# Twenty-two more identity products on TensorE in the first units of a fused attention, soft-MoE and squared-ReLU kernel

## The reference, cut to what matters

```python
# q, k, v: (8, 8, 576, 64); pool = 8, so 72 pooled keys per head
k_p = k.reshape(B, H, Sp, pool, D).mean(axis=3)
v_p = v.reshape(B, H, Sp, pool, D).mean(axis=3)
scores = scale * np.matmul(q, k_p.transpose(0, 1, 3, 2))
attn = softmax(scores)                      # over the 72 keys
x = (attn @ v_p) rearranged to (4608, 512)
logits = x @ phi                            # 32 slots
slot_out = per expert: relu((softmax(logits, 0).T @ x) @ w1) @ w2
x = softmax(logits, 1) @ slot_out
h = maximum(x @ w_in, 0);  out = (s * h * h + b) @ w_out
```

## Time and profile before

| | |
|---|---|
| median of 3 runs | 648.23 us |
| profiled execution | 652.14 us, span 650.3 us |
| busy in the span | PE 97%, DVE 74%, ACT 69%, POOL 19% |
| mean granted clock of PE | 0.986 of full speed |
| HBM | 70.32 MB read, 9.44 MB written |

### The profile page before, as it was taken

The page is one execution under the profiler, slowest core; times in us unless marked ns, Lnnn a source line. Parts: engine busy times, 40 slices in busy tenths (PEclk is TensorE's granted clock), DMA queues, the critical chain, the costliest instruction groups (busy, mean ns, idle before and its releaser), DMA issues.

```text
span 650.3 us, 16686 instructions
## 1 busy us (share of the span) xinstructions
PE 629.7 (97%) x6462; PEld 547.8 (84%) x6462; DVE 481.5 (74%) x796; ACT 448.9 (69%) x754; POOL 124.2 (19%) x126
## 2 busy tenths in 40 slices
PE   7799999999999999999999999999999999999996
PEld 7676776776763347889999999999999999999996
DVE  4888665665535739886888878888888887888876
ACT  1588766676522169996777777777777777777772
POOL 3787887542210010004000000000000000000001
PEclk9699989999999999999999999999999999999999
DMA  9968879386459980001000000000000000000001
GB/s 330 321 196 328 331 236 404 77 329 250 158 206 411 414 366 1 1 1 42 26 34 18 34 16 32 16 32 16 32 16 30 18 32 16 16 32 16 33 18 66
DMA packets 26005, 80.50 MB, mean 124 GB/s; under 512 B 6496, under 2 KB 14688, under 8 KB 23392
## 3 DMA queue, kind: packets, MB, share of 16 engines
q1 hardware_dynamic: 25952, 79.76, 32.9%
HBM read 70.32 MB, written 9.44 MB: 123 GB/s over the span
## 4 chain that ended last, share of the span: by engine, by line
PE 89%; DVE 3%; DMA 2%; POOL 2%; issue 2%; ACT 1%; DVEq 0%; ACTq 0%; POOLq 0%
PE bank L1999 16%; PE bank L2010 16%; PE bank L2000 16%; PE bank L1904 5%; PE bank L1772 5%; PE bank L1725 2%; PE bank L1751 2%; PE bank L1927 2%; PE bank L1631 2%; PE bank L1934 2%; PE bank L1930 2%; PE bank L1864 2%; PE bank L1840 2%; PE bank L1663 2%; DMA kvbuf<-in_v_dram 2%
## 5 line engine op out<-in xcount | busy, mean ns | idle before, releaser
L1388 DVE TENSOR_TENSOR lo_sb<-a_sb,hi_sb 128x896 fp32r<-128x896 f32 x128 | 140.1, 1094 | 57.2 <-PE bank L2010 55.5
L1053 ACT ACTIVATE hi_sb<-a_sb 128x896 fp32r<-128x896 f32 x128 | 122.2, 955 | 77.1 <-PE bank L2000 74.8
L1999 PE MATMUL bank<-w_hi,hi_sb 128*128 128x256 f32 x381 | 96.9, 283 | 0.0
L2000 PE MATMUL bank<-w_lo,hi_sb 128*128 128x256 f32 x381 | 96.9, 283 | 0.0
L1038 ACT ACTIVATE a_sb<-r_sb 128x512 f32<-128x512 f32 x144 | 91.1, 632 | 6.4
L2010 PE MATMUL bank<-w_hi,lo_sb 128*128 128x256 f32 x381 | 87.1, 283 | 0.0
L1031 ACT ACTIVATE r_sb<-bank 128x512 f32<-128x512 f32 x144 | 83.6, 580 | 0.1
L1999 PEld LDWEIGHTS bank<-w_hi,hi_sb 128*128 128x128 f32 x381 | 73.2, 192 | 0.0
L2000 PEld LDWEIGHTS bank<-w_lo,hi_sb 128*128 128x128 f32 x381 | 73.2, 192 | 0.0
L864 POOL TENSOR_TENSOR pu_sb<-pu_sb,logits 128x256 f32<-128x256 f32 x1 | 0.7, 740 | 334.5 <-DVE x_sb L1446 334.5
L1999 PE MATMUL bank<-t_early,hi_sb 128*128 128x256 f32 x256 | 64.3, 283 | 0.0
(11 more groups left out here) (213 smaller groups left out, 1333.0 us busy)
## 6 DMA issues: line engine op xcount, KB each, us to landing
early_third<-in_moe_w_dram SPq DMA_DIRECT2D x5, 2048.0 KB, 11.5
kvbuf<-in_k_dram SPq DMA_DIRECT2D x12, 768.0 KB, 5.6
kvbuf<-in_v_dram SPq DMA_DIRECT2D x12, 768.0 KB, 6.1
out_dram<-o_sb SPq DMA_DIRECT2D x36, 256.0 KB, 2.3
qbuf<-in_q_dram SPq DMA_DIRECT2D x8, 1024.0 KB, 7.9
early<-in_moe_w_dram SPq DMA_DIRECT2D x4, 2048.0 KB, 9.9
late<-in_moe_w_dram SPq DMA_DIRECT2D x3, 2048.0 KB, 14.3
after_last<-in_moe_w_dram SPq DMA_DIRECT2D x2, 2048.0 KB, 8.2
```

Source lines behind the costliest of these rows:

```text
L1053: act.activation(hi_sb[:, n % 2, :], a_sb[:, n % ARING, P:2 * CH], ACT.Copy).then_inc(hi_ready, 1)
L1388: dve.tensor_tensor(lo_sb[:, n % 2, :], a_sb[:, n % ARING, P:2 * CH], hi_sb[:, n % 2, :].bitcast(F32), ALU.subtract).then_inc(lo_ready, 1)
L1999: pe.matmul(acc, hi, rhs_hi, start=(k == 0 and (at == AT1 or at % 2 == 1)), stop=False, skip_group_check=True)
L2000: last = pe.matmul(acc, hi, rhs_lo, start=False, stop=False, skip_group_check=True)
```

## The change

`START_WARM` becomes four numbers in place of one. The first stands where the 7 products stood, behind the turn of the first keys. The others stand in steps 0, 1 and 2 of PE's loop, behind the turn of the queries (and in step 0 behind the turns of keys). 7 become 12 + 3 + 10 + 4 = 29.

```diff
-    START_WARM = 7
+    START_WARM = (12, 3, 10, 4)
...
             turn_keys(0, 0, 0)
-            for _ in range(START_WARM):
-                pe.matmul(bank[A_B[0]][:, 0:P], ident[:, :], ident[:, :], start=True, stop=True)
+            def fill_start(times):
+                for _ in range(times):
+                    pe.matmul(bank[A_B[0]][:, 0:P], ident[:, :], ident[:, :], start=True, stop=True)
+
+            fill_start(START_WARM[0])
...
                 if n == 0:
                     turn_keys(0, 1, 0)
                     turn_keys(0, 2, 0)
+                if n < GP:
+                    fill_start(START_WARM[1 + n])
```

## The result

The changed kernel is slower. Its median is 651.75 us over twelve executions on the chip, that of before 648.02 us over twelve beside it; the ratio is 1.0051, with a 95% interval of 1.003 to 1.0071, so it loses 3.3 us (2 to 4.6). I had forecast 646.4 us, 0.3% faster.

A forecast was written before the change was run, and what follows sets the result against it. PE, busy for 97% of the span, was taken as the bound; a full clock in front was to bring the chain's 50.78 us to 48.95, 1.8 us off the median of 648.23: 646.4 us, range 644.5 to 648.3.

The forecast's parts named there:

- What bounds the kernel, and the clock: PE, busy 97% of the span; filling its early holes should keep the clock full past 14.5 us, to about 21.
- The products themselves cost nothing: Front of PE's order: the 22 added products fit in existing waits at no cost; uncovered, 5.5 us at full clock.
- The gain at the load of values: DVE's first key group of the second pair starts at 26.15 us; SP's load of values leaves at 31.65, not 33.50.
- The sum: 50.78 becomes 48.95, 1.8 us less.: Chain's turn of weights on PE comes 1.8 us earlier, own range 1.2 to 2.3; forecast with both clock variants 62%.
- the four groups that each ends in "nothing": Behind first keys 5 products, before first scores 3, first values 10, second values 4: each said to cost nothing.
- the first rival: Late clock fall near 89.5 us moves: gone, 644.7 us (10%), or one more fall or instruction wait, 648.1 us (12%).
- The half clock: Third rival: clock half through the ten and four products in front, 1.9 us slower, 650.1 us; 8%.
- The late fall of the clock: Half clock from about 89.5 to 93 us disappears, gaining 1.7 us more, 3.5 in all: 644.7 us; 10%.

The follow-up runs named there:

- thin: Changed kernel with its 22 added products only one column wide, the first 7 kept: same instructions, next to no array work; 653.91 us, ratio 1.0085.
- held loads: Two 2 MB loads held until the queries of unit 30 are turned: ratio 0.9971 in the kernel before, 0.9995 changed, 0.9958 in the wide one, 1.0011 thin.
- the changed kernel run again: The changed kernel measured once more without any edit, beside the kernel before: 651.77 us, ratio 1.0048.
- the wide one: Changed kernel's front work as products of up to 512 columns, 4 instructions more than the kernel before instead of 88: 647.05 us, ratio 0.9991.
- The four comparisons at an equal place of the code: Warm against cold front at the same or 4 instructions' different code place: 0.09% and 0.34 to 0.37% with loads unmoved, 0.13% and 0.16% with them held.
- the displaced kernels: Kernels with 88 instructions more than before, changed and thin: ratios 1.0051, 1.0048 and 1.0085; with the two loads held 0.9995 and 1.0011.
- the held kernel before: The kernel before with only the two 2 MB loads held back: 646.20 us, ratio 0.9971.
- all four kernels of the table: Before, the wide one, changed and thin, each without and with held loads: ratios 1, 0.9991, 1.0051 and 1.0048, 1.0085; held 0.9971, 0.9958, 0.9995, 1.0011.

## Why the prediction was wrong

*What bounds the kernel, and the clock.* Right. The clock stayed full from before 9 us on; the fall at 14.5 and the return at 28 us are gone, in all eight profiles with the work of 29 products in front. What I did not see is that the cold stretch of before is not the same in every execution: two profiles with a cold front have it for 13.7 us (before, thin), two for 6.8 (both with held loads).

*The products themselves cost nothing.* Right as to the array: the first three groups ended before what stood behind them was released (11.9 against 12.62, 18.4 against 18.84 us), and the fourth ran up to the turn of values at 21.65, behind which the scores waited 0.24 us for DVE anyway.

*The gain at the load of values.* Right in mechanism and size: I had the first group of keys at 26.15 behind its load, it was at 26.00; the load of values at 31.65, it left at 31.46; the chain at 48.95, it was 49.20. PE has a new wait of 0.88 us for its own instructions at 40.6 on this chain; in the changed kernel run again it is missing, and the turn begins at 48.53.

*"The sum: 50.78 becomes 48.95, 1.8 us less."* This is the step that failed, and with it the line of the four groups that each ends in "nothing". I priced the 22 products by the array's time and by the waits that hide it. I had no term for what they are as code: 88 instructions that shift everything behind them. The trace had what was needed to suspect it. PE had five waits for its own instructions, 4.2 us together, one of them in the earlier trace rows with a fall of the clock behind it. I named this as half of the first rival, at 12%, and priced it at one more fall of 1.7 us, just what the front gains; that the change itself displaces the code of all later units had no price. The thin kernel measured the missing term at 5.5 us, the changed kernel against the wide one at 3.7 us: two to three times the gain.

*The other rivals.* The half clock, which was to bring the slower result, did not happen: the kernel is slower with a full clock. The late fall of the clock did go in the profiled execution, whose span shrank by 3.3 us where that rival had 3.5; taken alone, this trace would have confirmed a forecast that the median refutes.

*What the warm front is worth at the end.* The four comparisons at an equal place of the code give 0.09 to 0.37%, 0.6 to 2.4 us. Each rests on two ratios with intervals of 0.2 to 0.3% to either side, so 1.8 us is compatible with them and not confirmed by them. One reason for less is in the traces: I measured the gain against an execution with the long cold stretch. The turn of weights of the chain begins at 48.12 to 49.20 us in the eight profiles with the warm front, at 50.65 and 50.78 in the two with the long cold stretch, and at 49.65 and 50.28 in the two with the short one.

*What stays open.* Neither profiled execution of the changed kernel was a long one, so what makes its median 3 to 4 us longer than these was not seen. What speaks for longer holes is that their places are fixed and their length is not (1.01, 1.28, 2.38 us at the same boundary), and that moving two loads gives back 0.5 to 0.75% in the displaced kernels. For falls of the clock behind the holes speaks the one at 118 us in the held kernel before, and the executions' mean clocks: those of the changed kernel run again with 652 us and more have 0.991 to 0.997, those with 648 and less 0.998 or 0.999. A mean of 0.994 is an estimated 7.8 us at half clock in 650, up to 3.9 us of work. How the two share the 5 us between a short and a long execution is not settled. Nor is it known why before gains from held loads by more than its hole at 153 us, what the 0.4% are that 88 instructions cost with the loads held, or how far the code behind the attention units matters. The 37 packets are not the whole program: in the profile before none begins between 370 and 604 us, and how PE comes by its code there the profile does not say. A displacement by exactly 256 instructions, which should bring back the places of before, wasn't tried.

## What to carry to other kernels

In a program written out without loops, every instruction added on PE moved all later places at which PE can run out of code. When the gain looked for is a few microseconds, look at the waits for its own instructions first, and at what the DMA engines carry there: products of 512 columns give PE the same work in about a quarter of the instructions, and a large load with slack can be issued later: all four kernels of the table ran 0.3 to 0.75% shorter for it. One profiled execution can show a gain in every row and still belong to a kernel whose median is worse; a displaced kernel without the work, and the work without the displacement, tell the two apart.

## What the hardware showed that I had not expected

PE stopped for 2.38 us for its own code, in a stretch of 4 us in which one packet of it and 1.69 MB of data went through the DMA engines. The packet took 0.91 us; it had left late. With the two loads elsewhere, the same boundary caused no wait at all in either kernel. In every trace such a wait stands after 256 k + 193 records of PE and ends 1.2 to 1.6 us behind the packet.

The same front, instruction for instruction, was at half clock for 13.7 us in one profiled execution and for 6.8 in another.

Identity products of one column on 32 columns of weights took about 0.1 us each (ten records in 0.48 us at full clock), and in the thin kernel 22 of them did not keep the clock up: it was half from about 14 us on, with a mean of 0.86 over the first 50 us, as before. With held loads both kernels had 0.93.
